# The low half of a split weight against the 64 remaining rows of x: one 128-row matmul per chunk, or two 64-row array tiles per pair of chunks

## What is computed

```python
w = softmax(weight_gen, over the 7 taps)             # batch, seq, 8 heads, 7
x = sum over k of w[..., k] * x_padded[s + k]         # 8192 x 192
h = x @ moe_w_in;  r = np.maximum(h, 0.0);            y = (r * r) @ moe_w_out
h = y @ moe2_w_in; g = h / (1 + np.exp(-1.702 * h));  out = g @ moe2_w_out
```

## Time and profile before

| | |
|---|---|
| time, median of 3 runs | 1256.75 us (1256.33 to 1257.18) |
| span of the profiled execution | 1255.6 us |
| PE busy | 1207.4 us (96%) |
| PE weight loads busy | 1000.5 us (80%) |
| DVE busy | 831.9 us (66%) |
| ACT busy | 615.6 us (49%) |
| POOL busy | 479.6 us (38%) |
| mean granted TensorE clock | 0.993 of full speed (2.4 GHz) |
| chain that ended last | PE 93%, DVE 3%, the rest 1% each or less |

### The profile page before, as it was taken

How to read it: one execution, slowest core, us unless ns; L and a number is a source line. 1 busy time by engine, 2 the same in 40 slices (tenths; PEclk the granted TensorE clock), 3 DMA queues, 4 the chain that set the end, 5 groups by cost and what they waited for, 6 DMA issues and landing times.

```text
span 1255.6 us, 15052 instructions
## 1 busy us (share of the span) xinstructions
PE 1207.4 (96%) x5456; PEld 1000.5 (80%) x5456; DVE 831.9 (66%) x706; ACT 615.6 (49%) x616; POOL 479.6 (38%) x249
## 2 busy tenths in 40 slices
PE   1679999999999999999999999999999999999998
PEld 1568888888888888888888888888888888888886
DVE  5888757576675766657576675857667586664553
ACT  1456454545545454454545545454554545445443
POOL 6856408062360905317071450806226080530000
PEclk9899999999999999999999999999999999999999
DMA  6230010010101001010010101001010100100000
GB/s 189 64 116 2 1 44 0 0 44 0 44 0 44 0 0 44 0 44 0 8 36 0 44 0 44 0 0 44 0 44 0 41 3 0 44 0 13 1 11 15
DMA packets 10493, 30.77 MB, mean 25 GB/s; under 512 B 882, under 2 KB 5106, under 8 KB 10352
## 3 DMA queue, kind: packets, MB, share of 16 engines
q1 hardware_dynamic: 10480, 30.60, 7.6%
HBM read 24.30 MB, written 6.29 MB: 24 GB/s over the span
## 4 chain that ended last, share of the span: by engine, by line
PE 93%; DVE 3%; POOL 1%; issue 1%; ACT 1%; DMA 1%; SPq 0%; POOLq 0%; ACTq 0%
PE hidden L611 45%; PE acc L623 9%; PE acc L627 9%; PE acc L625 9%; PE acc L624 9%; PE acc L626 9%; PE hidden L667 1%; DVE g_hi L526 1%; DMA window<-x 1%; DVE g_lo L533 1%; PE hidden L665 1%; PE hidden L656 1%; PE hidden L658 1%; POOL attn L293 1%; POOL term L270 0%
## 5 line engine op out<-in xcount | busy, mean ns | idle before, releaser
L611 PE MATMUL hidden<-xin,win 128*128 128x512 f32 x2560 | 627.5, 392 | 6.9 <-DVE xin L543 6.6
L611 PEld LDWEIGHTS hidden<-xin,win 128*128 128x128 f32 x2560 | 480.2, 189 | 106.5 <-DVE xin L543 4.3
L533 DVE TENSOR_TENSOR g_lo<-gate,g_hi 128x1024 fp32r<-128x1024 f32 x256 | 428.3, 1673 | 149.4 <-ACT g_hi L422 145.0
L413 ACT ACTIVATE first<-hidden 128x1024 f32<-128x1024 f32 x256 | 263.1, 1028 | 356.6 <-PE hidden L611 355.3
L526 DVE CAST g_hi<-gate 128x1024 fp32r<-128x1024 f32 x128 | 137.0, 1071 | 191.2 <-PE acc L627 185.7
L270 POOL TENSOR_TENSOR attn<-window,probs 128x768 f32<-128x768 f32 (+1 forms) x16 | 24.2, 1512 | 602.7 <-DVE probs L513 596.9
L422 ACT ACTIVATE g_hi<-gate 128x1024 fp32r<-128x1024 f32 x128 | 135.8, 1061 | 203.6 <-DVE gate L530 203.6
L270 POOL TENSOR_TENSOR term<-window,probs 128x768 f32<-128x768 f32 (+1 forms) x96 | 209.8, 2192 | 10.4 <-POOL attn L293 9.8
L623 PE MATMUL acc<-g_hi,wout 128*128 128x512 f32 x512 | 200.6, 392 | 12.0 <-DVE g_lo L533 12.0
L627 PE MATMUL acc<-g_lo,wout 128*128 128x512 f32 x512 | 200.0, 391 | 0.0
L624 PE MATMUL acc<-g_lo,wout 128*128 128x512 f32 x512 | 200.0, 391 | 0.0
(11 more groups left out here) (53 smaller groups left out, 383.6 us busy)
## 6 DMA issues: line engine op xcount, KB each, us to landing
window<-x SPq DMA_DIRECT2D x14, 960.0 KB, 5.0
out<-work SPq DMA_DIRECT2D x16, 384.0 KB, 2.5
work<-moe_w_out SPq DMA_DIRECT2D x8, 384.0 KB, 3.4
work<-moe_w_in SPq DMA_DIRECT2D x4, 512.0 KB, 7.1
work<-moe_w_in SPq DMA_DIRECT2D x8, 256.0 KB, 4.2
probs<-weight_gen SPq DMA_DIRECT2D x1, 1568.0 KB, 15.4
window<-x SPq DMA_DIRECT2D x2, 384.0 KB, 12.4
window<-x SPq DMA_DIRECT2D x2, 283.5 KB
```

The costliest lines, as they stand in the source:

```text
L413: nc.scalar.activation(first[:, s.k, :], hidden_of(s), func, scale=scale).then_inc(first_done, 1)
L533: nc.vector.tensor_tensor(g_lo[:, s.k, :], gate[:, s.k, :], g_hi[:, s.k, :], ALU.subtract).then_inc(g_ready, 1)
L611: last = nc.tensor.matmul(hidden[:, s.slot, c, :], w[:, wi, cols], xt[:, xi, :], start=m == 0, stop=m == len(parts) - 1)
```

## The change

The matmul with `W_REST_LO` goes from each chunk, and with it the lo by lo product of the remaining rows. In its place each pair of chunks gets two matmuls of 64 contraction rows: one takes weights and x from partitions 0 to 63 and adds into chunk 0's bank, the other takes them from partitions 64 to 127 and adds into chunk 1's bank. They sit behind the eight full matmuls of the pair. Their weights are a new tile `tail` (partitions 0 to 63: lo of chunk 0 of the pair, partitions 64 to 127: lo of chunk 1), and the second needs the hi of x's rest in partitions 64 to 127: a new plane `X_TWIN`, which ScalarE copies once per group and layer. The lo of a "rest" piece becomes two subtracts of 64 partitions x 512 elements in place of one of 128 x 1024.

```diff
-        win = [sb(f"win{l}", [P, 4, F], F32R) for l in (RELU2, GELU)]
-        W_HI, W_LO, W_REST_HI, W_REST_LO = range(4)
+        win = [sb(f"win{l}", [P, 3, F], F32R) for l in (RELU2, GELU)]
+        W_HI, W_LO, W_REST_HI = range(3)
+        tail = [sb(f"tail{l}", [P, PAIRS, P], F32R) for l in (RELU2, GELU)]
-        xin = [sb(f"xin{l}", [P, 3, N], F32R) for l in (RELU2, GELU)]
-        X_HI, X_REST, X_LO = range(3)
+        xin = [sb(f"xin{l}", [P, 4, N], F32R) for l in (RELU2, GELU)]
+        X_HI, X_REST, X_LO, X_TWIN = range(4)
...
+        def lo_ops(q):
+            return 2 if pieces[q][0] == "rest" else 1
...
+            if kind == "rest":
+                cols = slice(1024 * part, 1024 * part + 1024)
+                raw = raw.rearrange("p (j c n) -> p j c n", c=2, n=P)
+                hi = win[layer][:, W_REST_HI, cols].rearrange("p (j c n) -> p j c n", c=2, n=P)
+                for c, rows in enumerate((slice(0, HALF), slice(HALF, P))):
+                    if alone is not None and alone + c:
+                        eng.wait_ge(done, alone + c)
+                    eng.tensor_tensor(tail[layer][rows, 4 * part:4 * part + 4, :], raw[rows, :, c, :],
+                                      hi[rows, :, c, :], ALU.subtract).then_inc(done, 1)
+                return
...
@@ GpSimd, lo_piece
-                split_piece_lo(nc.gpsimd, q).then_inc(piece_lo_pool, 1)
+                before = sum(lo_ops(r) for r in BY_POOL if r < q)
+                split_piece_lo(nc.gpsimd, q, piece_lo_pool, before)
+                if pieces[q][0] == "rest":
+                    pool.wait_ge(piece_lo_pool, before + 2)
@@ ScalarE, step xT, behind the copy of line 429
+                    nc.scalar.activation(xin[s.x][HALF:P, X_TWIN, :], hidden[HALF:P, s.slot, 1, :],
+                                         ACT.Copy).then_inc(x1_twin, 1)
@@ ScalarE, step split, behind the copy of line 440
+                    act.wait_ge(rest_done, s.g + 1)
+                    nc.scalar.activation(xin[s.x][HALF:P, X_TWIN, :], rest,
+                                         ACT.Copy).then_inc(x2_twin, 1)
@@ VectorE, step xT, ahead of the subtract of line 543
+                    dve.wait_ge(x1_twin, s.g + 1)
@@ TensorE, hidden_product
-                    parts = ((W_HI, X_HI), (W_HI, X_LO), (W_LO, X_HI), (W_REST_HI, X_REST),
-                             (W_REST_LO, X_REST))
+                    parts = ((W_HI, X_HI), (W_HI, X_LO), (W_LO, X_HI), (W_REST_HI, X_REST))
...
+                low, high = slice(0, HALF), slice(HALF, P)
+                nc.tensor.matmul(hidden[:, s.slot, 0, :], tail[s.layer][low, s.j, :],
+                                 xt[low, X_REST, :], start=False, stop=True)
+                last = nc.tensor.matmul(hidden[:, s.slot, 1, :], tail[s.layer][high, s.j, :],
+                                        xt[high, X_TWIN, :], start=False, stop=True)
                 last.then_inc(slot_ready, 1)
@@ TensorE, do, first pair of a group
+                        if s.layer == GELU:
+                            pe.wait_ge(x2_twin, s.g + 1)
```

More of the change, by code:

```diff
@@ L199, in build @@
         x1_ready = sem("x1_ready")
+        x1_twin = sem("x1_twin")
+        x2_twin = sem("x2_twin")
         upper_copied = sem("upper_copied")
@@ L224, in build @@
         SOFTMAX_AFTER = {1: 1, 3: 2, 7: 3, 9: 4}
+        def lo_ops(q):
+            return 2 if pieces[q][0] == "rest" else 1
         def piece_split(eng, q):
             for mine, done in ((True, piece_lo_pool), (False, piece_lo)):
-                count = sum((r in BY_POOL) == mine for r in range(q + 1))
+                count = sum(lo_ops(r) for r in range(q + 1) if (r in BY_POOL) == mine)
                 if count:
@@ L251, in split_piece_hi, with split_piece_lo @@
             return nc.scalar.activation(dst, piece_raw(q), ACT.Copy)
-        def split_piece_lo(eng, q):
+        def split_piece_lo(eng, q, done, alone=None):
             kind, layer, part = pieces[q]
             raw = piece_raw(q)
+            if kind == "rest":
[8 more added lines that the diff above has]
+                return
             if kind == "out":
@@ L259, in split_piece_lo @@
                 eng.tensor_tensor(w[:, :, 2 * P:2 * D], raw[:, :, 0:P], w[:, :, 0:P], ALU.subtract)
-                return eng.tensor_tensor(w[:, :, D:2 * P], raw[:, :, P:D], w[:, :, P:D], ALU.subtract)
-            hi, lo = (W_HI, W_LO) if kind == "in" else (W_REST_HI, W_REST_LO)
+                eng.tensor_tensor(w[:, :, D:2 * P], raw[:, :, P:D], w[:, :, P:D],
+                                  ALU.subtract).then_inc(done, 1)
+                return
             cols = slice(1024 * part, 1024 * part + 1024)
-            return eng.tensor_tensor(win[layer][:, lo, cols], raw, win[layer][:, hi, cols], ALU.subtract)
+            eng.tensor_tensor(win[layer][:, W_LO, cols], raw, win[layer][:, W_HI, cols],
+                              ALU.subtract).then_inc(done, 1)
         def attention_mul(eng, g, k, dst, row0, t0, t1):
@@ L517, in lo_piece @@
                 dve.wait_ge(piece_hi, q + 1)
-                split_piece_lo(nc.vector, q).then_inc(piece_lo, 1)
+                split_piece_lo(nc.vector, q, piece_lo)
             def do_pair(s, opened):
@@ L605, in hidden_product @@
                 w, xt = win[s.layer], xin[s.x]
-                for c in range(2):
-                    cols = slice((2 * s.j + c) * P, (2 * s.j + c + 1) * P)
-                    parts = ((W_HI, X_HI), (W_HI, X_LO), (W_LO, X_HI), (W_REST_HI, X_REST),
-                             (W_REST_LO, X_REST))
+                chunks = [slice((2 * s.j + c) * P, (2 * s.j + c + 1) * P) for c in range(2)]
+                for c, cols in enumerate(chunks):
+                    parts = ((W_HI, X_HI), (W_HI, X_LO), (W_LO, X_HI), (W_REST_HI, X_REST))
                     for m, (wi, xi) in enumerate(parts):
-                        last = nc.tensor.matmul(hidden[:, s.slot, c, :], w[:, wi, cols], xt[:, xi, :],
-                                                start=m == 0, stop=m == len(parts) - 1)
+                        nc.tensor.matmul(hidden[:, s.slot, c, :], w[:, wi, cols], xt[:, xi, :],
+                                         start=m == 0, stop=False)
+                low, high = slice(0, HALF), slice(HALF, P)
[3 more added lines that the diff above has]
+                                        xt[high, X_TWIN, :], start=False, stop=True)
                 last.then_inc(slot_ready, 1)
```

## The result

The changed kernel takes 1305.71 us (median of 4 runs, 1305.15 to 1306.53) against 1256.61 for the kernel before: 49 us slower, ratio 1.039 (95% interval 1.038 to 1.041). The span of its profiled execution is 1304.7 us.

A forecast was written before the change was run, and what follows sets the result against it. TensorE's 512-column matmuls at 227 ns were taken as the bound; the profiled span 1255.6 - 42.7 = 1212.9 us, plus 1.15 from span to median, gave 1214 us. Range 1198 to 1305 us, the overlap case alone 1198 to 1230.

The forecast's parts named there:

- What bounds the kernel: From 87 us on, PE sets the time: number of 512-column matmuls times 227 ns; the other engines wait for it.
- The price of the form: Per pair on TensorE: two full matmuls (454 ns) become overlapping 64-row tiles, saving 172 ns, x 248 = 42.7 us.
- the emptying of the array: Rival at each pair's two changes of form: array empties first; chance 0.17 with weights ready, 0.17 with loads exposed.
- Rival 1: Array empties at each change of form: 1282 us with weights ready, 1332 or 1377 with load exposed; chances 0.17 each.
- the two cases: Emptying with weights ready, 1259 to 1305 us, and with loads exposed, 1305 to 1380 us; chance 0.17 each.
- a gap of 0.17 us or more: Sign of being wrong: such a gap ahead of the first tile or behind the second would show the array emptying.
- The threshold: One change of form costing more than 113 ns, half of 227, turns the sign; below that, 1200 to 1257 us.
- The drain rule: Skill page's statement that changing the tiling mode, not just the tile, drains TensorE; cited for Rival 1, without a price.
- The second tile's delay: Second tile of a pair starts 55 ns after the first, taken between 0 and 110 ns from the transposes' loads.
- Copies, waits, weight pieces: ScalarE's 32 added copies (19 us), the new waits and the halved weight subtracts were taken to cost 0.
- The opening: Start of the kernel, up to the wait ending at 87.30 us: change taken as 0, 2 us either way.
- Another engine as the bound: Rival: ACT or DVE limits the shorter pair, 4.36 us in place of 4.54; given no chance of its own.

## Why the prediction was wrong

- **What bounds the kernel.** Right: PE's waits stayed the same five (the two small ones read from the earlier trace rows are one, seen at the load and at the matmul), and the time moved by pairs times the change per pair, 248 x 0.203 = 50 us.
- **The price of the form.** This step failed. The sum 454 - 227 - 55 = 172 ns saved per pair has no term for the change of form: I chose overlap, which was right, and put the emptying of the array among the rivals with 0.34 in all, because no row of before shows another form. The runs show 0.20 us per change, 0.40 per pair (1412.12 against 1256.09, two changes and a slot), where the sum had nothing. The sign was thereby wrong: 203 ns lost per pair instead of 172 saved. What I held against the rival, transposes that follow without a gap, says nothing of it, since they keep the form 128\*128.
- **Rival 1's own sum** was near. Its two prices were 165 ns for a change with weights ready and 265 with the load exposed, 1282 and 1332 us. Measured: the load is exposed, at the 0.10 us that the earlier trace rows gave, but it starts 0.09 to 0.10 us after the successor's due time and not 0.165, before the recorded end of the last matmul. That is 0.20 per change, and 2 x 200 - 227 = 173 ns x 248 = 43 us would make 1300. The second tile, with the slower pace behind it, adds 7.5 us, which this rival's sum left out, and carries the time to 1306. The range ended at 1305, because I had cut between the two cases and left the upper one out. The sign of being wrong that I had named, a gap of 0.17 us or more, was set too high as well: in the starts the gap is 0.09, and the load shows in the duration of 0.50. The threshold was right: above 113 ns per change it is slower.
- **The drain rule.** The Trainium skill (page "TensorEngine Tiling (Array Packing)", section "Key Properties") says that a change of tiling mode drains the TensorE and a change of tile doesn't. The traces agree in both halves: 0.32 us from the tiles' start to the full form's load against 0.10 us to the next tiles' loads, in the run with four tiles. I had it as a rival of its own and gave it no more weight than the absence of rows; with no row that spoke against it, it should have weighed more.
- **The second tile's delay.** I took 55 ns between 0 and 110; it is 3 or 4 ns, loads included. The end taken from the earlier trace rows was the wrong one: those loads follow one another on the same rows, and with both tiles on the same rows they are 0.11 apart here too. Together with the slower pace the second tile costs 30 ns.
- **Copies, waits, weight pieces at nothing.** Right: 1255.43 against 1256.52 us with everything but the form. The opening, taken as 0 with 2 us either way, gave 1.2 us back.
- **Another engine as the bound.** I gave it no chance by counting latencies. At 18 slots per pair it costs some 42 us (1185.7 against 1144), so at the forecast's 19.2 slots part of the 43 us gain might have been lost too. I counted the 8.6 us up to a pair's output product; the slot behind `xT` is wanted 2.9 us after its hidden product ends (290.62 to 293.52 before). The count also left out that in VectorE's queue a slot's `gate` stands behind the `g_lo` of the pair ahead, and that the same subtract takes 1.2 us in one place and 2.0 in another, as here in the changed kernel. No run has that pace, so how much stays open.

```profile
287.52 1.96 DVE L560 TENSOR_TENSOR g_lo<-gate,g_hi 128x1024 fp32r<-128x1024 f32 x1 [1.19 <-ACT g_hi L444]
...
296.99 1.23 DVE L560 TENSOR_TENSOR g_lo<-gate,g_hi 128x1024 fp32r<-128x1024 f32 x1 [1.35 <-ACT g_hi L444]
```

## What to carry to other kernels

A smaller matmul form has to be paid twice, going in and coming back, and in a stream that otherwise hides every load that was 0.20 us each, nearly a slot of 0.227. Mixed into such a stream it pays only where a visit replaces clearly more than two slots by one: here two tiles per visit lose, and four would only break even (a visit of 0.89 us, from the run with four tiles, against 0.907 for four full matmuls; no run makes that exchange). Before work is taken off the bounding engine, read which waits for the others are only just covered, as the 0.58 us behind `xT`: with two slots per pair fewer, 113 us by count, 42 of them did not arrive.

## What the runs showed of the hardware that I had not expected

- Two 64-row loads for different halves of the array start 3 or 4 ns apart; on the same half they are 0.11 us apart (632.59 and 632.70), as the 128-row loads of the earlier trace rows are (0.10 to 0.11).
- The load for the other form starts about 0.07 us before the recorded end of the matmul ahead of it, going in and coming back, in every run with tiles (here 633.75 against some 633.82). The profile models these ends, so whether the array is empty by then is not shown; that the load is held back is.
- Behind a restart the 512-column matmuls of the full form can keep to 229 to 232 ns instead of 227 for some ten matmuls, at full granted clock (1.00 from 90 us on); it was slowest behind the upper tile alone, and absent behind the lower tile alone. No cause found.
